# Attention state scan, softmax-weighted layer and routed experts on one core: half slots moved among the slots, product steps and one addition moved in VectorE's order

## The chip, the cores and the metric

The kernel runs on one core of one Trainium2 chip. The metric is the device time in microseconds (us) of one execution; lower is better. A kernel is timed several times, and its median is quoted. One further reading is the profiled execution, of which the trace gives every instruction.

## The reference

Three stages follow each other. Shapes: batch B = 4, heads H = 8, sequence S = 768, head dimension D = 48, so 3072 tokens of 384 numbers; all in float32.

```python
# 1: a linear recurrence over the sequence, per batch and head, with a complex decay a
S_re, S_im = a_re*S_re - a_im*S_im + outer(k[t], v[t]),  a_re*S_im + a_im*S_re
y[t] = q[t] @ S_re
# 2: x is y laid out as (3072, 384)
h = x @ w_in                       # (3072, 1024)
solu = h * softmax(h)
x = layernorm(solu) * g_ln @ w_out # (3072, 384)
# 3: two of eight experts for each token, by noisy logits
out[token] += weight[token, k] * (relu(x[token] @ w1[e]) @ w2[e])   # w1: 384x1024, w2: 1024x384
```

## The kernel before

**First phase, tokens.** Stages 1 and 2 and the routing of stage 3 run in 24 steps n = 4c + b, one for each chunk c of 128 positions (six) and batch b (four). `over_tiles` calls one `body(c, b, n)` for every engine; in it the engines work on different tiles at once: VectorE (DVE) prepares tile n, the matmul engine (PE) works on tile m = n-1 of the recurrence, on i = n-2 of the hidden product (L1624) and on j = n-3 of the second product (L1672). Each engine runs its own list in order, and semaphores join the lists. What is multiplied is split into a high and a low part, so each product of the layers is three matmuls.

In DVE's body the places that matter stand in this order: the low part `zl` (L1343), the maximum (L1369), the product with the softmax (L1388), the addition of a new term to the running state (L1394, semaphore `w_added`), then `weigh` and `k_products` (kp, L1236), the low part `xl` of the new tile (L1412, semaphore `xt_lo`), `q_products` (qp, L1227). Between them lie seven numbered places, `fill(0)` to `fill(6)`. Each call issues as many steps of the cumulative products of the decays (`product_op`, L1112 to L1140) as the table `FILLS` gives for this place: row `FILLS[0]` serves c = 0 and `FILLS[1]` serves c = 1 to 4, with one tuple for each b. The first 45 of 63 steps of a chunk are chain steps (L1112, L1117, L1120 in turn), the other 18 carry steps (four of L1134, then L1137 and L1140). `norm` scales the decays of a later chunk.

PE's list for step n is: transposes of kp (L1554), hidden product (L1624, 24 matmuls, which wait for `xt_lo` of the step before), `a_mm` (L1646, which waits for `zl` and qp), the new state term (L1661), the second product (L1672), L1684, transposes, L1690, the gate logits (L1704, which wait for `w_added` of the tile of this step), transposes of z.

**Second phase, experts.** The routed rows are cut into 31 slots: 25 whole slots of 256 rows and 6 half slots of 128. The tuple `HALF_SLOTS` says which of the 31 are halves; `table_row` maps a slot to its row of the routing table, `give_block` and `units` read the tuple too. A slot s loads `w1` and `w2` of its expert (1.5 MB each, SyncE's queue SP), splits them in high and low (ScalarE, L825 and L830, then DVE, L1241 and L1247), and computes eight blocks f: hidden product (L1563), relu (ScalarE `hh`, L1032), low part (DVE `hl`, L1509), output product (L1764). A half slot needs the same weights and half the matmuls, and it is ordered in another way (`half_slot`; its output product is L1792).

The output is accumulated in memory, so the slots form a chain. `partial(s)` on GpSimd (POOL) gathers the rows of `out` into `prev` (L731) once the rows that slot s-1 scattered have landed (`y_sent`). `give(s)` on DVE adds the slot's product to them (`yo`, L1502), and POOL's `give` scatters them back (L740). DVE carries out `give(s-1)` inside slot s, behind block f = `give_block(s-1)`, or near the start of a half slot: `give_block` is 4 in the slot right behind a half slot, then 3, 2, and 1 from there on. Everything of DVE behind `give` waits with it, the `hl` of the next blocks included.

SP's loop loads, for each s in turn, `mine` of slot s+3 (after `y_sent` of slot s-3) and then the weights of slot s+1.

Of the kernel before, what the change touches and what calls it, by code (L numbers as in the profile page):

```python
# [31 lines left out]
MAXS = NTOK // CAP  # L32
WHOLE, HALVES = 25, 6
SLOTS = WHOLE + HALVES
HALF_SLOTS = (3, 8, 12, 17, 21, 26)
ROWS = (E + 1) * REGION
NG = 3
LINE = 16
# [18 lines left out]
def is_half(s):  # L57

    return s in HALF_SLOTS


def table_row(s):

    return WHOLE + HALF_SLOTS.index(s) if is_half(s) else s - sum(t < s for t in HALF_SLOTS)

# [6 lines left out]
def units_upto(s, step=1):  # L72

    return sum(units(t) for t in range(s, -1, -step))


def give_block(s):

    return max([GIVE] + [4 - (s - t) for t in HALF_SLOTS if t <= s])


def steps(s):

    return sum(2 if is_half(t) else FC for t in range(s))


def wait(eng, sem, value):

    if isinstance(value, int) and value <= 0:
        return  # L90
    eng.wait_ge(sem, value)
# [29 lines left out]
def solu_moe_program(nc, q, k, v, a_re, a_im, w_in, w_out, g_ln, w_gate, w_noise, noise, w1, w2, out):  # L121
# [3 lines left out]
    with ExitStack() as ctx:  # L125
# [246 lines left out]
        def part(t, q):  # L372
            return t[:, :, :, q % 2, :, :].rearrange("p g h x i -> p (g h) (x i)")
# [10 lines left out]
        def mag(q, s_):  # L384

            return cum_part(q, s_) if q < 4 else magnitude[:, s_]

        def spare(h_, g):

            return slice(64 * h_ + D, 64 * h_ + 64), slice(64 * h_ + 16 * g, 64 * h_ + 16 * (g + 1)), g  # L390

        def spread_first(eng, h_):

            t = rcs[0].rearrange("p n h c x i -> p n (h c x i)")
            for from_, to, g in SPARE[NG * h_:NG * (h_ + 1)]:
                eng.dma_start(t[to, NG], t[from_, g]).then_inc(rc_spread, 16)

        SPARE = tuple(spare(h_, g) for h_ in range(2) for g in range(NG))
        FILLS = (((0, 0, 0, 0, 0, 0, 0), (0, 0, 0, 0, 0, 0, 16), (4, 1, 6, 1, 2, 3, 17), (4, 9, 0, 0, 0, 0, 0)),
                 ((6, 1, 9, 1, 2, 0, 3), (12, 1, 3, 1, 2, 1, 0), (8, 1, 2, 1, 3, 0, 4), (2, 0, 0, 0, 0, 0, 0)))  # L400
        assert all(sum(map(sum, x)) == CHAIN + CARRY for x in FILLS)

        def gated(group):
# [11 lines left out]
        def apart(eng, *waits):  # L415


            for s_, x in waits:
                wait(eng, s_, x)
                eng.sem_inc(passed[eng.engine], 1)  # L420
# [339 lines left out]
        def _(act):  # L760
# [282 lines left out]
            def half_slot(s, par, more):  # L1043

                s0, k = steps(s), 2 * HALF_SLOTS.index(s)

# [29 lines left out]
        def _(dve):  # L1076
# [100 lines left out]
            def norm(q):  # L1177
                ar, ai = ars[q // 2 % 2], ais[q // 2 % 2]
                s_ = mag(q, 0)
                dve.wait_ge(sc_done, q + 1)  # L1180
                V.tensor_tensor(part(ar, q), part(ar, q), s_, ALU.mult).then_inc(an_done, 1)
                halves = [t.rearrange("p (g h) x -> p g h x", h=2) for t in (part(ai, q), s_)]
                low, high = ([t[:, :, h_, :] for t in halves] for h_ in range(2))
                V.scalar_tensor_tensor(out=low[0], in0=low[0], scalar=-1.0, in1=low[1], op0=ALU.mult,
                                       op1=ALU.mult).then_inc(an_done, 1)
                V.tensor_tensor(high[0], high[0], high[1], ALU.mult).then_inc(an_done, 1)
# [105 lines left out]
            def body(c, b, n):  # L1292
# [4 lines left out]

                fills = FILLS[c > 0][b] if prep else (0,) * 7
                made = [sum(map(sum, FILLS[c > 0][:b]))]

                def fill(place):

                    for k_ in range(fills[place]):
                        product_op(c + 1, made[0] + k_)
                    made[0] += fills[place]
# [74 lines left out]
                if has(i):  # L1380
                    s0 = 4 * i
                    par = i % 2
                    dve.wait_ge(solu_step, s0 + 1)
                    V.reciprocal(esum[:, 2:3], esum[:, 1:2]).then_inc(solu_step, 1)
                    fill(3)

                    apart(dve, (solu_step, s0 + 2), (rstd_done, 2 * (i - 1)))
                    V.scalar_tensor_tensor(out=z[:], in0=z[:], scalar=esum[:, 2:3],  # L1388
                                           in1=bank[:, 4:6, :].rearrange("p b x -> p (b x)"), op0=ALU.mult,
                                           op1=ALU.mult, accum_out=mv[par][:, 0:1]).then_inc(solu_step, 1)  # L1390
                if B <= m < LIVE:

                    apart(dve, (w_mm, m + 1), (state_step, 3 * (m - B + 1)), (wide_done, 2 * (m - B + 1)))
                    V.tensor_tensor(state[:, m % B].rearrange("p s n e -> p (s n e)"),  # L1394
                                    state[:, m % B].rearrange("p s n e -> p (s n e)"),
                                    bank[:, 6, 0:2 * NP * D], ALU.add).then_inc(w_added, 1)
                fill(4)
                if c == 0 and b == 2:
                    norm(2 * c + 4)
                if b == 3 and c + 2 < C:  # L1400
                    norm(2 * c + 5)
                if b == 3 and prep:
# [22 lines left out]
                if b == 3 and prep:  # L1425
                    newton(2 * c + 2)

            over_tiles(dve, body)


# [119 lines left out]
        def _(pe):  # L1550
# [191 lines left out]
            def expert_hidden(s, par, f):  # L1742
# [3 lines left out]
                if f == 0 and s > 0 and is_half(s - 1):  # L1746
                    pe.wait_ge(row_done, 2 * HALF_SLOTS.index(s - 1) + 1)
                else:
# [29 lines left out]
            def half_turn(s, par, part):  # L1778
                if part == 0:
                    wait(pe, y2_evac, units_upto(s - 2))  # L1780
                pe.wait_ge(row_done, 2 * HALF_SLOTS.index(s) + part + 1)
                for k_ in range(4):
# [99 lines left out]
```

## Time and profile before

| | us |
|---|---|
| median of 3 runs | 1122.89 |
| the three runs | 1119.02, 1122.89, 1128.33 |
| the profiled execution, its own time | 1128.33 |
| its span in the trace | 1126.6 |

The profile covers the execution with 1128.33, the longest of the three; the time around its span is 1.7 us. The page gives busy time by engine, the span in 40 slices, the queues, the chain that ended last and the costliest groups. A row of a timeline reads: start, duration, engine, line, operation, output and inputs, shape, how many merged, and in brackets how long the engine was idle before it and who released it. PEclk is the granted clock of the matmul engine, 1.00 for 2.4 GHz and 0.50 for 1.2 GHz.

### The profile page before, as it was taken

How to read it: one execution, taken by the hardware profiler on the slowest of the kernel's cores; microseconds unless marked ns; L12 is line 12 of the kernel's file. 1: busy time of each engine (PE TensorE's matmuls, PEld its weight loads, DVE VectorE, ACT ScalarE, POOL GpSimd, SP SyncE). 2: the span in 40 equal slices, each digit the busy share in tenths (PEclk: the TensorE clock that was granted, in tenths of full speed). 3: DMA queues.
4: the chain of work that ended last, by engine and by line, in shares of the span. 5: the costliest groups of instructions: out<-in, count | busy, mean ns of one | idle time of the engine just before them, and what ended most of it. 6: DMA issues, size and time to landing. Idle time of an engine off the chain costs nothing.

```text
span 1126.6 us, 20986 instructions
## 1 busy us (share of the span) xinstructions
PE 994.2 (88%) x7460; PEld 924.6 (82%) x7460; DVE 845.6 (75%) x1572; ACT 640.4 (57%) x1081; POOL 423.9 (38%) x389
## 2 busy tenths in 40 slices
PE   0447899999999999999946999999999999999996
PEld 0246798888888888979846999999899999999996
DVE  5799999889899898645554777676766776677672
ACT  6744666856865855635433565565555656455551
POOL 4013133245353443434533334344344434434432
PEclk9868799999999999999967999999999999999998
DMA  9521131241221212221407867776676677667720
GB/s 238 195 94 33 35 102 37 63 93 49 52 92 51 50 37 57 51 57 30 134 15 276 278 220 248 269 249 235 245 262 241 227 265 274 215 244 280 261 72 20
DMA packets 84823, 167.43 MB, mean 149 GB/s; under 512 B 17417, under 2 KB 56544, under 8 KB 84720
## 3 DMA queue, kind: packets, MB, share of 16 engines
q1 hardware_dynamic: 72336, 137.60, 37.9%
q0 software_dynamic: 12288, 28.39, 7.0%
q8 instruction: 60, 0.98, 0.4%
q14 instruction: 43, 0.35, 0.1%
q10 hardware_dynamic: 96, 0.10, 0.0%
HBM read 146.46 MB, written 20.74 MB: 148 GB/s over the span
## 4 chain that ended last, share of the span: by engine, by line
PE 39%; DMA 12%; issue 6%; DVE 4%; ACT 2%; POOL 1%; POOLq 0%; DVEq 0%; another core or an unknown queue 0%; ACTq 0%; SPq 0%
PE bank L1563 12%; PE bank L1764 10%; DMA prev<-out,mine 8%; PE bank L1624 4%; PE bank L1672 4%; DMA out<-yo,mine 3%; PE bank L1554 3%; PE bank L1792 2%; DVE yo L1502 2%; PE bank L1646 1%; PE bank L1684 1%; DVE w1l L1241 1%; ACT z L991 1%; POOL prev L731 0%; POOL out L740 0%
## 5 line engine op out<-in xcount | busy, mean ns | idle before, releaser
L1032 ACT ACTIVATE hh<-bank 128x256 fp32r<-128x256 f32 x200 | 76.8, 384 | 219.9 <-PE bank L1563 210.7
L1563 PE MATMUL bank<-sxh,w1h 128*128 128x256 f32 x600 | 172.2, 287 | 2.1 <-issue 2.1
L1563 PE MATMUL bank<-sxh,w1l 128*128 128x256 f32 x600 | 170.2, 284 | 0.0
L1563 PE MATMUL bank<-sxl,w1h 128*128 128x256 f32 x600 | 169.9, 283 | 0.0
L1509 DVE SCALAR_TENSOR_TENSOR hl<-bank,hh 128x256 fp32r<-128x256 f32 x200 | 84.5, 423 | 91.7 <-ACT hh L1032 85.2
L1764 PE MATMUL bank<-w2h,hh 128*128 128x384 f32 x400 | 136.3, 341 | 5.5 <-DVE hl L1509 5.5
L740 POOL DMA_INDIRECT out<-yo,mine x56 | 67.0, 1197 | 193.4 <-DVE yo L1502 185.8
L1764 PE MATMUL bank<-w2l,hh 128*128 128x384 f32 x400 | 134.9, 337 | 0.0
L1764 PE MATMUL bank<-w2h,hl 128*128 128x384 f32 x400 | 134.8, 337 | 0.0
L1247 DVE TENSOR_TENSOR w2l<-raw,w2h 128x768 fp32r<-128x768 f32 x124 | 117.4, 961 | 20.5 <-ACT w2h L830 20.0
L1241 DVE TENSOR_TENSOR w1l<-raw,w1h 128x1024 fp32r<-128x1024 f32 x93 | 112.4, 1221 | 20.7 <-ACT w1h L825 19.8
L1563 PEld LDWEIGHTS bank<-sxh,w1h 128*128 128x128 f32 x600 | 114.1, 190 | 2.5 <-issue 2.5
L1563 PEld LDWEIGHTS bank<-sxh,w1l 128*128 128x128 f32 x600 | 114.8, 191 | 0.0
L1563 PEld LDWEIGHTS bank<-sxl,w1h 128*128 128x128 f32 x600 | 114.5, 191 | 0.0
L731 POOL DMA_INDIRECT prev<-out,mine x56 | 74.3, 1327 | 101.4 <-DMA out<-yo,mine 84.3
L830 ACT ACTIVATE w2h<-raw 128x768 fp32r<-128x768 f32 x124 | 101.6, 837 | 0.0
L825 ACT ACTIVATE w1h<-raw 128x1024 fp32r<-128x1024 f32 x93 | 96.3, 1051 | 0.0
L668 POOL TENSOR_SCALAR_AFFINE_SELECT at<-at 128x1024 f32<-128x1024 f32 x24 | 28.8, 1201 | 177.7 <-ACT at L939 177.7
L1624 PE MATMUL bank<-wi_hi,xh 112*128 112x512 f32 x192 | 80.5, 419 | 3.0 <-issue 3.0
L1764 PEld LDWEIGHTS bank<-w2h,hh 128*128 128x128 f32 x400 | 76.4, 191 | 7.4 <-DVE hl L1509 3.5
L939 ACT ACTIVATE at<-bank 128x1024 f32<-128x1024 f32 x24 | 24.6, 1023 | 94.6 <-PE bank L1646 94.6
L1624 PE MATMUL bank<-wi_lo,xh 112*128 112x512 f32 x192 | 78.1, 407 | 0.0
(237 smaller groups left out, 2564.1 us busy)
## 6 DMA issues: line engine op xcount, KB each, us to landing
raw<-in_w SPq DMA_DIRECT2D x62, 1536.0 KB
ar<-in_a_re SPq DMA_DIRECT2D x6, 768.0 KB, 4.8
turn<-in_a_im SPq DMA_DIRECT2D x6, 768.0 KB, 6.9
qk<-in_q SPq DMA_DIRECT2D x48, 96.0 KB, 2.4
qk<-in_k SPq DMA_DIRECT2D x48, 96.0 KB, 2.5
out<-wide SPq DMA_DIRECT2D x9, 512.0 KB, 12.3
vt<-in_v SPq DMA_DIRECT2D x24, 192.0 KB, 2.6
xs<-x SPq DMA_DIRECT2D x24, 192.0 KB, 2.6
```

What stands on the lines that cost most here:

```text
L731: nc.gpsimd.indirect_dma_start(prev[par][:, u, :], None, out, bass.IndirectOffsetOnAxis(ap=mine[k][:, u, 0:1], axis=0), bounds_check=NTOK ...
L740: nc.gpsimd.indirect_dma_start(out, bass.IndirectOffsetOnAxis(ap=mine[k][:, u, 0:1], axis=0), yo[par][:, u, :], None, bounds_check=NTOK - ...
L825: nc.scalar.activation(w1h[par][:, cc, :], raw1[par][:, cc, :], ACT.Copy).then_inc(w1_hi, 1)
L830: nc.scalar.activation(w2h[par][:, W2C * j:W2C * (j + 1), :], raw2[par][:, W2C * j:W2C * (j + 1), :], ACT.Copy).then_inc(w2_hi, 1)
L1032: nc.scalar.activation(hh[:, f % NH, :], bank[:, f % 2, 0:CAP], ACT.Relu).then_inc(hh_done, 1)
L1241: V.tensor_tensor(w1l[par][:, cc, :], raw1[par][:, cc, :], w1h[par][:, cc, :].bitcast(F32), ALU.subtract).then_inc(w1_lo, 1)
L1247: V.tensor_tensor(w2l[par][:, cut, :], raw2[par][:, cut, :], w2h[par][:, cut, :].bitcast(F32), ALU.subtract).then_inc(w2_lo, 1)
L1509: V.scalar_tensor_tensor(out=hl[:, f % NH, :], in0=bank[:, f % 2, 0:CAP], scalar=0.0, in1=hh[:, f % NH, :].bitcast(F32), op0=ALU.max, op1= ...
L1563: ins = MM(dst, stationary[a_](cc), moving[b_](cc), start=(n_ == 0), stop=(n_ == len(terms) - 1))
L1624: ins = MM(bank[:, 4 + half, :], (xh, xl)[a_][0:PR, cc, :], (wi_hi, wi_lo)[b_][0:PR, cc, 512 * half:512 * half + 512], start=(k_ % (3 * NP ...
L1672: ins = MM(bank[:, 0, 0:DM], (zh, zl)[a_][:, cc, :], (wo_hi, wo_lo)[b_][:, cc, :], start=(k_ == 0), stop=(k_ == len(x_terms) - 1))
L1764: ins = MM(bank[:, Y_BANK[par] + u, 0:DM], a_[:, f % NH, rows], b_[par][:, f, :], start=(f == 0 and k_ == 0), stop=(f == FC - 1 and k_ == 2))
```

## The change

Three edits:

1. `HALF_SLOTS` goes from (3, 8, 12, 17, 21, 26) to (3, 8, 13, 18, 23, 28). The distances between half slots were 5, 4, 5, 4, 5 and are 5, 5, 5, 5, 5; behind the last half slot came four whole slots and now come two.
2. `FILLS` moves product steps from place 6 (behind `q_products`) to place 5 (between `k_products` and `xl`): nine in c = 0, b = 2; three in b = 0 and four in b = 2 of c = 1 to 4.
3. The addition of the state (L1394) moves behind `fill(4)`, and behind a `norm` that exists in a step where there is no such addition.

```diff
-HALF_SLOTS = (3, 8, 12, 17, 21, 26)
+HALF_SLOTS = (3, 8, 13, 18, 23, 28)
...
-        FILLS = (((0, 0, 0, 0, 0, 0, 0), (0, 0, 0, 0, 0, 0, 16), (4, 1, 6, 1, 2, 3, 17), (4, 9, 0, 0, 0, 0, 0)),
-                 ((6, 1, 9, 1, 2, 0, 3), (12, 1, 3, 1, 2, 1, 0), (8, 1, 2, 1, 3, 0, 4), (2, 0, 0, 0, 0, 0, 0)))
+        FILLS = (((0, 0, 0, 0, 0, 0, 0), (0, 0, 0, 0, 0, 0, 16), (4, 1, 6, 1, 2, 12, 8), (4, 9, 0, 0, 0, 0, 0)),
+                 ((6, 1, 9, 1, 2, 3, 0), (12, 1, 3, 1, 2, 1, 0), (8, 1, 2, 1, 3, 4, 0), (2, 0, 0, 0, 0, 0, 0)))
...
+                fill(4)
+                if c == 0 and b == 2:
+                    norm(2 * c + 4)
                 if B <= m < LIVE:
 
                     apart(dve, (w_mm, m + 1), (state_step, 3 * (m - B + 1)), (wide_done, 2 * (m - B + 1)))
                     V.tensor_tensor(state[:, m % B].rearrange("p s n e -> p (s n e)"),
                                     state[:, m % B].rearrange("p s n e -> p (s n e)"),
                                     bank[:, 6, 0:2 * NP * D], ALU.add).then_inc(w_added, 1)
-                fill(4)
-                if c == 0 and b == 2:
-                    norm(2 * c + 4)
```

## Rows read from the trace of the kernel before

**Rows 1.** Page, part 2: PE's granted clock in the 40 slices of the span.

```profile
PEclk9868799999999999999967999999999999999998
```

**Rows 2.** Windows by stage: bounds, length, busy of PE, PEld, DVE, ACT, POOL, clock, DMA.

```profile
400.00:480.00 80.00, 77.04 (x698) 69.11 (x697) 64.44 (x145) 46.47 (x86) 35.53 (x36) 1.00 0.20 49
...
598.00:1116.00 518.00, 506.41 (x3465) 496.87 (x3466) 359.77 (x507) 283.27 (x465) 201.82 (x164) 0.98 0.68 237
```

**Rows 3.** Waits of PE in the second phase (598 to 1126 us): total, times, longest.

```profile
PE bank L1764 <- DVE hl L1509: 5.5, 5, 1.8
```

**Rows 4.** Windows between the starts of the xg transposes of successive slots.

```profile
692.71:710.28 17.57, 17.57 (x127) 17.54 (x126) 11.73 (x18) 9.55 (x17) 7.33 (x5) 1.00 0.72 257
710.28:729.43 19.15, 18.02 (x127) 17.68 (x126) 13.81 (x21) 10.03 (x17) 8.78 (x8) 1.00 0.71 253
729.43:741.36 11.93, 11.93 (x80) 11.50 (x78) 9.23 (x13) 7.72 (x13) 5.91 (x5) 1.00 0.67 232
741.36:757.01 15.65, 15.40 (x103) 14.70 (x102) 12.50 (x17) 9.68 (x16) 6.15 (x5) 1.00 0.60 211
792.15:807.70 15.55, 13.75 (x80) 13.11 (x79) 11.44 (x16) 8.21 (x14) 7.02 (x6) 0.89 0.62 220
...
952.50:971.88 19.38, 17.24 (x102) 16.34 (x101) 12.39 (x17) 9.77 (x16) 9.61 (x8) 0.91 0.64 225
1007.02:1026.63 19.61, 18.09 (x128) 17.68 (x127) 14.67 (x22) 10.04 (x17) 8.78 (x8) 1.00 0.68 244
```

**Rows 5.** Timeline of DVE: the accumulation yo in slots 7 and 11.

```profile
725.55 1.14 DVE L1502 SCALAR_TENSOR_TENSOR yo<-bank,mine,prev 128x384 f32<-128x384 f32 x2 [1.72 <-DMA prev<-out,mine]
...
792.85 1.14 DVE L1502 SCALAR_TENSOR_TENSOR yo<-bank,mine,prev 128x384 f32<-128x384 f32 x2 [2.82 <-DMA prev<-out,mine]
```

**Rows 6.** Windows of about 3.3 us behind PE's waits in slots 11 and 7.

```profile
796.10:799.40 3.30, 3.30 (x16) 3.30 (x15) 2.15 (x4) 0.10 (x1) 1.14 (x1) 0.50 0.32 119
...
728.40:731.80 3.40, 3.40 (x24) 3.36 (x25) 2.71 (x4) 0.90 (x3) 1.46 (x2) 1.00 0.53 194
```

**Rows 7.** Timeline of DVE in the last slot, slot 30.

```profile
1102.59 1.13 DVE L1502 SCALAR_TENSOR_TENSOR yo<-bank,mine,prev 128x384 f32<-128x384 f32 x2
...
1106.47 0.42 DVE L1509 SCALAR_TENSOR_TENSOR hl<-bank,hh 128x256 fp32r<-128x256 f32 x1 [1.69 <-ACT hh L1032]
...
1116.76 1.14 DVE L1502 SCALAR_TENSOR_TENSOR yo<-bank,mine,prev 128x384 f32<-128x384 f32 x2 [1.41 <-PE bank L1764]
```

**Rows 8.** Windows of half a microsecond: the last one with DMA before 1118 us.

```profile
1112.00:1112.50 0.50, 0.50 (x6) 0.50 (x5) 0.00 (x0) 0.10 (x1) 0.00 (x0) 1.00 0.07 1
```

**Rows 9.** Timeline of DVE, steps 16 and 18: xl, chain steps, carry steps.

```profile
402.62 0.69 DVE L1412 TENSOR_TENSOR xl<-bank,xh 112x512 fp32r<-112x512 f32 x1
...
407.40 0.36 DVE L1112 TENSOR_TENSOR ct<-cum,ar 128x192 f32<-128x192 f32 x1
...
408.47 0.36 DVE L1112 TENSOR_TENSOR ct<-cum,ar 128x192 f32<-128x192 f32 x1
...
439.70 0.69 DVE L1412 TENSOR_TENSOR xl<-bank,xh 112x512 fp32r<-112x512 f32 x1 [0.73 <-ACT xh L997]
...
441.51 1.96 DVE L1134 TENSOR_TENSOR turn<-cum 128x384 f32<-128x384 f32 x4
```

**Rows 10.** Timeline of PE: first matmul of the hidden product behind steps 16 and 18.

```profile
403.61 0.48 PE L1624 MATMUL bank<-wi_hi,xh 112*128 112x512 f32 x1
...
440.96 0.48 PE L1624 MATMUL bank<-wi_hi,xh 112*128 112x512 f32 x1
```

**Rows 11.** Waits of PE from 100 to 560 us: total, times, longest.

```profile
PE bank L1554 <- DVE kp L1236: 13.3, 12, 2.4
```

**Rows 12.** Timeline of step 6: the state addition, the gate logits, the kp transposes.

```profile
188.87 0.54 DVE L1394 TENSOR_TENSOR state<-state,bank 128x384 f32<-128x384 f32 x1
...
189.52 0.81 PE L1704 MATMUL bank<-wg,x2t 128*128 128x16 f32 x6
...
193.06 1.10 PE L1554 MATMUL bank<-ident,kp 128*128 128x128 f32 x8 [1.55 <-DVE kp L1236]
```

## The prediction

> **What bounds the kernel now.** I read the windows by stage first. From 598 to 1116 us, the expert slots, PE is busy for 506.41 of 518 us, DVE for 359.77 [rows 2]: the slots run at PE's pace, and what can be won is PE's 11.6 idle microseconds and what half clock costs. In the first phase PE and DVE are both nearly full; from 400 to 480 us PE is busy 77.04 of 80 and DVE 64.44 [rows 2]. The clock by slice is a full 9 almost throughout the second half and lower at the start and at the seam (the 6 and 7 in the middle) [rows 1].
>
> Next, which wait of PE ends last in the slots. Its list of waits names the low part `hl`, 5.5 us in five waits of 1.8 at most [rows 3]. The page's means hide where they are, so I took windows between the starts of the xg transposes, which mark the slots. A whole slot without a wait takes 17.57 us, the way into a half slot 11.93 and out of it 15.65. Five windows are longer: 19.15 and 19.61 for a whole slot (slots 7 and 25), 15.55 and 19.38 around the half slots 12 and 21 [rows 4], and slot 16, which is of the kind of 7 and 25 and lies near them. Third, DVE's timeline says why `hl` is late: it stands behind `yo`, which waited 1.72 us in slot 7 and 2.82 us in slot 11 for the gather `prev` [rows 5]. So the chain through memory (yo, scatter, gather, yo) is what ends last there. Fourth, the granted clock behind these waits: behind PE's wait in slot 11 it is 0.50 for 3.3 us, behind that in slot 7 it stays 1.00 [rows 6].
>
> **Edit 1, the half slots.** A half slot is short, so the chain falls behind; `give_block` puts `give` at block 4 and takes it forward by one block a slot. In the three slots behind a half slot two successive gives are therefore one block, about 2.1 us, closer than a slot is long: 15.4 us. With a distance of 5 the slot ahead of the next half has its give at block 1 and loses 19.15 - 17.57 = 1.6 us (slot 7) or 19.61 - 17.57 = 2.0 us (slot 25) [rows 4]; I take 1.8 for each of the three (7, 16, 25). With a distance of 4 the half slot arrives one slot earlier, while the give is at block 2, and the chain has about 4 us less: 15.55 - 11.93 = 3.6 us lost around half slot 12, 19.38 - 15.65 = 3.7 around 21 [rows 4]. Of either, about 1.7 us is the stretch of 3.3 to 3.4 us at half clock (half of it is lost) [rows 6]. Before: 3 x 1.8 + 3.6 + 3.7 = 12.7 us. After: the slots 7, 12, 17, 22 and 27 each stand ahead of a half at distance 5: 5 x 1.8 = 9.0 us. Gain 3.7 us. Work and weights of a slot are the same wherever it stands; idle rows skip their transfers as before.
>
> The Trainium skill (TensorE: Matmul & The Clock Gate, HAM oscillation) says that waits for data between bursts of matmuls drop the clock and are paid again in slow matmuls. The trace agrees for slot 11, clock 0.50 behind the wait, and not for slot 7, clock 1.00 [rows 6]. By that rule each of five waits would have its price; that is the first rival below.
>
> **The end, which edit 1 also touches.** The last half slot was four slots from the end and is now two. So `give(29)` in slot 30 goes from block 1 to block 3. Now its yo starts at 1102.59; the `hl` of block 3 is at 1106.47 and yo would follow at about 1106.8, 4.2 us later [rows 7]. The gather for the last slot ends its transfers by 1112.5 [rows 8]; shifted by 4.2 this is 1116.7, and the last yo, which waits for both, starts at 1116.76 on PE's account [rows 7]. The cover of 4.2 us is used up to the last tenth, and the signal behind the last packet comes on top. Bounds: nothing, if the signal is quick, and 4.2 us, the whole shift. The nearest row is the half microsecond in which the traffic ends, so I stay near the low end and take 1.0.
>
> **Edit 2, product steps ahead of xl.** DVE's total is unchanged, and the steps keep their order; `xl` and `q_products` come later, and `zl` stays where it was. PE's hidden product waits for `xl`. Three chain steps take 408.47 - 407.40 = 1.07 us, four carry steps 1.96 us [rows 9]. In step 16 (c = 4, b = 0) `xl` ends at 403.31 and PE starts at 403.61 [rows 9, 10]; the closest that PE follows is about 0.1, so 0.2 us are cover and about 0.85 is a new delay. In step 18, `xl` was idle for 0.73 us, ends at 440.39, and PE starts at 440.96 [rows 9, 10]: 1.96 - 0.73 - 0.47 = 0.76 us. Between there and the end of c = 4 PE has no wait that could absorb it: together 1.6 us. In steps 4 to 14 the same delays, 0.7 to 1.8 us each, meet PE's waits for kp in the step behind: twelve of them, 13.3 us in all, 2.4 at most [rows 11]. kp stands ahead of the moved steps and is not later, so these waits shrink instead: nothing. In step 2 nine steps, some 3.3 us, go ahead of `xl`; PE waits there later for `zl` anyway. I take nothing, with 2 us as the other bound, for the clock was at half in parts of it. If all the cover were gone, eight delays of about 1.3 us would be 10 us; so all of edit 2 lies between 0 and 10. Queued behind the moved `q_products` is SP's load of the next q and k, which has a whole step of 19 us until it is used. No price.
>
> **Edit 3, the state addition.** It goes behind two chain steps (0.7 us), three carry steps (1.5 us) or none. DVE is not idle ahead of it, so nothing is won. PE's gate logits wait for it: in step 6 it ends at 189.41 and PE starts at 189.52 [rows 12], so a delay of 1.5 us reaches PE at once. Behind it PE waits 1.55 us for kp [rows 12], and kp is not later. The cover and the delay are equal within 0.1: 0 to 0.3 us over the five steps where the logits follow at once; I take nothing. Without that cover it would be 2 x 1.5 + 3 x 0.7 = 5.1 us.
>
> **Sum.** -3.7 + 1.0 + 1.6 = -1.1 us. Against the profiled execution that is 1128.33 - 1.1 = 1127.2 (span 1125.5); it was the longest of the three, 5.4 above the median. For the median, 1122.89 - 1.1 = 1121.8 us.
>
> **Rivals.**
>
> *The waits at distance 5 drop the clock too* (slower). Place: slots 7, 12, 17, 22, 27. Price: 1.7 us for each, 8.5 in all: -1.1 + 8.5 = +7.4, 1130.3 us. It outweighs the gain from the third slot on that does so. For it: PE's waits of 1.8 in slot 11 did it. Against: slot 7 did not [rows 6].
>
> *The slots no longer wait at all*: even distances let the chain recover, and all of 12.7 us come back: -12.7 + 2.6 = -10.1, 1112.8 us. For it: only the irregular ones lose 3.6. Against: slots 7 and 25 lose at distance 5 already [rows 4].
>
> *Edit 1 wins nothing*: the longer waits in slots 11 and 21 come from where the weight loads (237 GB/s on average [rows 2]) fall upon the gather, and they move to other slots. Then 0 + 2.6: 1125.5 us.
>
> *The cover in the first phase fails*: PE and DVE take turns as the one that is late, and delays add instead of being absorbed. Half of 10 + 5.1 on top: -1.1 - 1.6 + 7.5 = +4.8, 1127.7 us.
>
> *The first phase pays*: the 0.73 us idle ahead of `xl` is used, no delay reaches PE, the end has its cover: -3.7 - 0.7 = -4.4, 1118.5 us.
>
> **How the numbers follow.** The forecast has 0.45; the clock 0.10, no waits at all 0.08, nothing won 0.12, cover fails 0.12, first phase pays 0.13. The predicted time is 1121.8. The range takes in the forecast, nothing won, the cover failing and the first phase paying, with the spread of the three runs around the median (4 down, 5 up) as a reason not to be narrower: 1115 to 1128. Within 1% is 1111.7 to 1134.1, about what a measurement of this kernel can tell from no change; every case lies inside it, and the outer bounds of the unknown costs reach past it only when they add up. Faster by over 1%: 0.06, within 1%: 0.89, slower by over 1%: 0.05.
>
> **What would show each step right or wrong.** Windows between the xg transposes: all lengths 17.57, 11.93 and 15.65 but for slots 7, 12, 17, 22, 27 with 1.5 to 2.0 more, and none of 3.6 more; the clock at 1.00 from 620 us on. In slot 30 yo at block 3, and the last yo idle for `prev` instead of PE. In steps 16 and 18, the first L1624 about 0.1 us behind `xl` with steps L1112 or L1134 ahead of it; DVE's 0.7 us idle there gone; in steps 4 to 14 the waits for kp shorter by what the hidden product started late. I would be wrong if the end waits more than 2 us for `prev`, if the clock falls in more than one of the five slots, or if DVE is found idle for PE in c = 1 to 3 where it was not.

## The result and the profile after

| | us |
|---|---|
| before, median (19 runs) | 1125.29 (1119.02 to 1129.10) |
| after, median (19 runs) | 1132.55 (1125.47 to 1137.82) |
| ratio after to before | 1.0055, 95% interval 1.0038 to 1.0074 |
| the profiled execution of after, its own time and span | 1130.34, 1128.6 |

The change makes the kernel slower by 0.55%, 6.2 us (4.3 to 8.3). The forecast was -1.1 us. In absolute terms 1132.55 stands against the predicted 1121.8 and lies outside the stated range of 1115 to 1128; 2.4 of these 10.8 us are the kernel before itself, whose median is 1125.29 over 19 runs and was 1122.89 over the three known at the prediction. Differences below are the ratio's distance from 1 times about 1125 us, with its interval. The two profiled executions differ by only 2.0 us, so a trace shows where time goes but not how much it is on average; that is what the medians are for.

The windows by stage and around slot 27 of the changed kernel, to be read as [rows 2, 4]:

```profile
400.00:480.00 80.00, 77.49 (x670) 70.09 (x670) 61.82 (x145) 43.16 (x78) 28.18 (x30) 0.96 0.18 47
600.00:1117.00 517.00, 504.89 (x3465) 495.24 (x3466) 359.79 (x507) 282.97 (x465) 193.19 (x164) 0.98 0.68 238
1037.59:1061.92 24.33, 19.00 (x128) 18.53 (x127) 15.28 (x23) 10.02 (x17) 9.27 (x8) 0.90 0.60 210
1061.92:1074.72 12.80, 12.80 (x79) 12.37 (x78) 8.23 (x12) 7.72 (x13) 4.41 (x4) 0.93 0.52 175
...
1059.90:1063.80 3.90, 3.90 (x15) 3.80 (x16) 2.41 (x3) 0.00 (x0) 1.52 (x2) 0.50 0.37 110
```

From the first xg transposes to those of slot 30 pass 489.9 us (1090.36 - 600.49), before 490.7: in these two executions the slots last equally long, but the time is lost in other places. The third row runs from the transposes for slot 27 to those for half slot 28: 24.33 us where a slot takes 17.57. The slots 7, 12, 17 and 22 lose 1.70, 0.98, 0.62 and 1.13 us in the same trace; slot 27 loses 6.76, and the window behind it another 0.87 (12.80 where it takes 11.93), more than those four together. The last row shows the clock at 0.50 behind the wait, on both sides of the border between the two windows. PE's waits in the second phase, against [rows 3]:

```profile
PE bank L1764 <- DVE hl L1509: 7.9, 7, 4.8
```

One wait of 4.8 us is new. Its surroundings in the timelines of DVE, PE, POOL and SP:

```profile
1057.11 1.14 DVE L1502 SCALAR_TENSOR_TENSOR yo<-bank,mine,prev 128x384 f32<-128x384 f32 x2 [5.39 <-DMA prev<-out,mine]
...
1059.86 0.66 PE L1764 MATMUL bank<-w2h,hh 128*128 128x384 f32 x1 [4.80 <-DVE hl L1509]
...
1039.32 1.20 POOL L740 DMA_INDIRECT out<-yo,mine  x1 [6.74 <-DVE yo L1502]
1040.83 1.13 POOL L740 DMA_INDIRECT out<-yo,mine  x1 [0.31 <-issue]
1048.09 1.59 POOL L731 DMA_INDIRECT prev<-out,mine  x1 [6.13 <-DMA out<-yo,mine]
...
1026.78 0.36 SPq L564 DMA_DIRECT2D mine<-tags  x1
1027.96 0.38 SPq L554 DMA_DIRECT2D raw<-in_w  x1
...
1041.31 0.38 SPq L554 DMA_DIRECT2D raw<-in_w  x1
```

Read from the bottom: SP issues the 1.5 MB of w1 for slot 29 at 1041.31, while POOL is issuing slot 25's scatter (1039.32 to 1041.96). It is the first weight load that has no `mine` ahead of it: slot 30's `mine`, at 1026.78, was the last. POOL then waits 6.13 us behind the scatter's second issue until the rows have landed; in the other 28 waits of this kind in the trace it is 2.0 to 4.4 us, 2.44 in many. The two halves of the scatter part here: the one issued at 1039.32, ahead of the load, lands 2.8 us after its issue, the one issued at 1040.83 lands 6.4 us after it. The gather `prev` of slot 26 is issued that much later, yo in slot 27 waits 5.39 us for it, and PE 4.80. The Trainium skill (DMA: Bandwidth & Descriptors, Issuing engines are not separate DMA queues) says that transfers started by different engines run on the same DMA engines and interleave; the trace agrees: POOL's scatter, with SP's load issued beside it, is waited for 6.13 us and not 2.44.

In the first phase, PE's waits from 100 to 560 us, against [rows 11]:

```profile
PE bank L1624 <- issue: 12.2, 10, 4.3
PE bank L1704 <- issue: 8.5, 6, 3.8
PE bank L1554 <- DVE kp L1236: 6.2, 8, 2.2
```

Waits moved: those for kp went from 13.3 to 6.2 us, and the hidden product and the logits wait instead. All of PE's waits there add up to 28.0 us before and 30.0 after. At the end of the kernel:

```profile
1107.84 1.13 DVE L1502 SCALAR_TENSOR_TENSOR yo<-bank,mine,prev 128x384 f32<-128x384 f32 x2
...
1118.85 1.14 DVE L1502 SCALAR_TENSOR_TENSOR yo<-bank,mine,prev 128x384 f32<-128x384 f32 x2 [2.48 <-DMA prev<-out,mine]
```

The last yo now waits for `prev` and not for PE [rows 7]. From the transposes for slot 30 (1090.36; 1089.34 before) to it are 28.49 us, before 27.42: 1.1 us more.

### The profile page after: what moved, and what is told of

Its sections match the earlier page's. It is cut to its first block, busy times and chain, and to the rows that moved or that the text cites. A ratio compares the mean times of both kernels' runs of the same rounds, so it can differ in the third digit from the quotient of the medians.

```text
span 1128.6 us, 20986 instructions
## 1 busy us (share of the span) xinstructions
PE 992.8 (88%) x7460; PEld 923.3 (82%) x7460; DVE 842.6 (75%) x1572; ACT 639.6 (57%) x1081; POOL 402.6 (36%) x389
## 4 chain that ended last, share of the span: by engine, by line
PE 43%; DMA 10%; issue 6%; DVE 4%; ACT 2%; POOL 1%; POOLq 0%; DVEq 0%; ACTq 0%; SPq 0%
PE bank L1563 13%; PE bank L1764 10%; DMA prev<-out,mine 6%; PE bank L1624 5%; PE bank L1672 4%; PE bank L1554 3%; DMA out<-yo,mine 3%; PE bank L1792 2%; PE bank L1646 2%; DVE yo L1502 2%; PE bank L1684 2%; DVE w1l L1241 1%; ACT z L991 1%; POOL out L740 1%; ACT w1h L825 0%
## 5 line engine op out<-in xcount | busy, mean ns | idle before, releaser
L731 POOL DMA_INDIRECT prev<-out,mine x56 | 70.9, 1267 | 97.4 <-DMA out<-yo,mine 85.9
```

What stands on the lines that cost most here:

```text
L731: nc.gpsimd.indirect_dma_start(prev[par][:, u, :], None, out, bass.IndirectOffsetOnAxis(ap=mine[k][:, u, 0:1], axis=0), bounds_check=NTOK ...
```

## The experiments

Theory A: the loss is slot 27. SP's loop holds back the weights of slot s+1 by the wait of `load_mine(s + 3)`, for the scatter of slot s-3. From s = 28 on there is no `mine` left, and nothing keeps the load off a scatter. Before, that fell on the slots behind half slot 26, which have late gives (blocks 4 and 3); now it falls on slot 27, with its give at block 1. Theory B: the loss is in the first phase, where delays add instead of being absorbed.

### The three edits one by one

Edit 1 alone:

```diff
-HALF_SLOTS = (3, 8, 12, 17, 21, 26)
+HALF_SLOTS = (3, 8, 13, 18, 23, 28)
```

> Only the half slots move; the first phase is that of before. Theory A (the loss is in the last slots: the weight load of slot 29 starts unpaced while slot 25's scatter lands, and slot 27, now a slot with its give at block 1, waits for prev): +3 to +5 us against before, with one wait of PE of 3 to 5 us in slot 27 and the other slots 3 to 6 us cheaper than before together. Theory B (the loss is in the first phase, where delays add instead of being absorbed): -3 us or less, and no long wait in slot 27 beyond chance.

Measured: 1.0052 (1.0029 to 1.0076), +5.8 us. The long wait is there again, 4.70 us, with the load at 1038.29 and the scatter issued from 1036.29 on:

```profile
1038.29 0.38 SPq L554 DMA_DIRECT2D raw<-in_w  x1
...
1045.10 1.55 POOL L731 DMA_INDIRECT prev<-out,mine  x1 [6.16 <-DMA out<-yo,mine]
...
1056.74 0.66 PE L1764 MATMUL bank<-w2h,hh 128*128 128x384 f32 x1 [4.70 <-DVE hl L1509]
```

Edit 2 alone: the `FILLS` table of after in the kernel before.

> Only the product steps move to the place ahead of xl. Theory A: +1 to +2.5 us, what the trace of the changed kernel shows at the seam (600.49 against 598.62). Theory B: +5 us or more.

Measured: 1.0023 (1.0000 to 1.0046), +2.6 us (0 to 5.2).

Edit 3 alone: the addition behind `fill(4)` in the kernel before.

> Only the state addition moves behind the product steps of place 4. Theory A: within 1 us of before; PE's gate logits start later where they follow the addition, and the wait for kp behind them shrinks. Theory B: +2 us or more.

Measured: 0.9985 (0.9959 to 1.0011), -1.7 us (-4.6 to +1.2), no difference that is clear.

Edits 2 and 3 together: after, with the old half slots.

> The changed kernel with the old half slots: edits 2 and 3 together. From the two alone (+2.6 and -1.7): +0.9 us against before; by the prediction: +1.6 us. If the two edits hurt each other in the first phase (the cover of one used up by the other): +4 us or more.

Measured: 1.0001 (0.9976 to 1.0026), +0.1 us (-2.7 to +2.9). So the first phase costs 2.9 us at most and by the median nothing, and edit 1, with 5.8 us alone, carries the 6.2. Theory B falls.

### Holding the last loads back

```diff
                 if s + 3 < SLOTS:
                     load_mine(s + 3, (s + 3) % NM)
+                else:
+                    apart(sp, (y_sent, 16 * units_upto(s - NM + 3)))
                 load_w1(s + 1)
                 load_w2(s + 1)
```

> The changed kernel, with SyncE's queue waiting for the scatter of slots 25 and 26 before it loads the weights of slots 29 and 30, as the load of mine makes it wait in all slots before. Theory A: the wait of 4.8 us in slot 27 goes down to the 0.4 to 1.0 us of slots 12, 17 and 22, and the clock stays full: 5 to 8 us less than the changed kernel, so 0 to 2 us under before. Theory B: no change against the changed kernel, +6 us against before.

Measured: 1.0002 (0.9981 to 1.0023), +0.2 us against before, so 6.0 us less than the changed kernel (the intervals of the two, -2.1 to +2.6 and 4.3 to 8.3, do not meet). Slot 27 in its trace; the two added lines make every later line number two higher:

```profile
1042.65 0.38 SPq L554 DMA_DIRECT2D raw<-in_w  x1
...
1037.53 1.20 POOL L742 DMA_INDIRECT out<-yo,mine  x1 [7.68 <-DVE yo L1504]
1039.03 1.14 POOL L742 DMA_INDIRECT out<-yo,mine  x1 [0.31 <-issue]
1042.60 1.08 POOL L733 DMA_INDIRECT prev<-out,mine  x1 [2.43 <-DMA out<-yo,mine]
...
1053.73 0.41 PE L1766 MATMUL bank<-w2h,hh 128*128 128x384 f32 x1 [0.44 <-DVE hl L1511]
```

The load starts 5.1 us behind the scatter's first issue (1037.53), where in the changed kernel it was 2.0; POOL waits 2.43 us for the scatter, whose two halves each land 2.7 to 2.8 us after their issue, and PE waits 0.44 where it waited 4.80. The window of slot 27 (1034.84 to 1054.87) is still 2.5 us longer than 17.57, for PE waits 1.48 us near its start as well, at 1038.21; but the clock stays at 1.00.

The same with edit 1 alone, and with the kernel before:

> Edit 1 alone with the paced weight loads of slots 29 and 30; the first phase is that of before. This is the term of the prediction's sum by itself: -3.7 for the even distances and +1.0 for the end, so -2.7 us against before. If the even distances win nothing and only the unpaced load was wrong with edit 1: 0 to +1 us. If the pacing was not what took the loss away: +5 us, as edit 1 alone had.

Measured: 0.9994 (0.9975 to 1.0013), -0.7 us (-2.8 to +1.5).

> The kernel before with the same two paced loads. If the unpaced load only hurts where it meets a slot with its give at block 1 (slots 27 of the changed kernel), before gains nothing: within 1.5 us. If it hurts wherever it stands, 3 us or more less than before.

Measured: 1.0016 (0.9994 to 1.0038), +1.8 us (-0.7 to +4.3). Before gains nothing that is clear of noise. Its trace shows why nothing was to be won: the unpaced loads hold up the scatters there too, but the rows are needed later.

```profile
1040.39 0.38 SPq L554 DMA_DIRECT2D raw<-in_w  x1
...
1043.09 1.02 POOL L740 DMA_INDIRECT out<-yo,mine  x1 [7.14 <-DVE yo L1502]
...
1050.95 1.68 POOL L731 DMA_INDIRECT prev<-out,mine  x1 [4.93 <-DMA out<-yo,mine]
...
1056.17 0.38 SPq L554 DMA_DIRECT2D raw<-in_w  x1
...
1065.17 1.02 POOL L731 DMA_INDIRECT prev<-out,mine  x1 [5.83 <-DMA out<-yo,mine]
...
1072.72 1.14 DVE L1502 SCALAR_TENSOR_TENSOR yo<-bank,mine,prev 128x384 f32<-128x384 f32 x2 [0.96 <-DMA prev<-out,mine]
```

POOL waits 4.93 and 5.83 us for the scatters of slots 25 and 26. But the give of slot 26 stands at block 4 and its yo does not wait, that of slot 27 stands at block 3 and waits 0.96 us, and PE does not wait for it in the slots 26 to 29.

### The cause everywhere, and the give of slot 26 later

The kernel before, with the weights ahead of `mine` in SP's order:

```diff
-                if s + 3 < SLOTS:
-                    load_mine(s + 3, (s + 3) % NM)
                 load_w1(s + 1)
                 load_w2(s + 1)
+                if s + 3 < SLOTS:
+                    load_mine(s + 3, (s + 3) % NM)
```

> The kernel before, with SyncE's queue issuing the weights of slot s+1 ahead of mine of slot s+3 instead of behind it, so no weight load is held back by the scatter of slot s-3. If the order of the queue is what keeps weight loads off the scatter (theory A), every slot now meets what slot 27 of the changed kernel met: the gather prev is issued 5 to 6 us behind the scatter instead of 2.4, and the tight slots 7, 11/12, 16, 21 and 25 lose 4 to 7 us each: 15 to 25 us more than before. If slot 27's wait had another cause: within 3 us of before.

Measured: 1.0310 (1.0279 to 1.0341; four runs), +34.9 us, more than expected. The expectation's total did not follow from its own price: five places at 4 to 7 us are 20 to 35. In the trace these five lose 4 to 8 us each more than before, 30 together. Its windows around slots 7 and 25:

```profile
712.42:737.81 25.39, 18.99 (x127) 18.52 (x126) 15.53 (x23) 10.03 (x17) 9.16 (x8) 0.95 0.53 180
1034.04:1058.70 24.66, 19.62 (x128) 19.21 (x126) 14.70 (x22) 10.02 (x17) 8.74 (x8) 0.93 0.56 183
```

The scatter of slot 5 and the gather for slot 6, which yo in slot 7 needs, in its timelines of POOL and SP:

```profile
715.44 1.20 POOL L740 DMA_INDIRECT out<-yo,mine  x1 [4.64 <-DVE yo L1502]
...
717.43 0.38 SPq L554 DMA_DIRECT2D raw<-in_w  x1
...
724.33 1.47 POOL L731 DMA_INDIRECT prev<-out,mine  x1 [6.25 <-DMA out<-yo,mine]
```

And its waits of PE in the second phase, against [rows 3]:

```profile
PE bank L1764 <- DVE hl L1509: 20.6, 8, 4.6
...
PE bank L1792 <- DVE hl L1528: 8.8, 2, 4.4
```

The slots 7 and 25, 19.15 and 19.61 us before [rows 4], now lose 7.8 and 7.1 us, what slot 27 lost in the changed kernel. PE's waits for `hl` grow by 22.0 us (20.6 + 8.8 against 5.5 and 1.9 for the half slots before); the clock at half behind most of them costs more. The load at 717.43 stands 2.0 us behind the scatter's first issue, as in slot 27. So the cause of slot 27 is the order of SP's queue, and it can be made at will.

Edit 1 alone, unpaced, with slot 26's give at block 3:

```diff
-    return max([GIVE] + [4 - (s - t) for t in HALF_SLOTS if t <= s])
+    return max([3 if s == 26 else GIVE] + [4 - (s - t) for t in HALF_SLOTS if t <= s])
```

> Edit 1 alone, loads unpaced, but the give of slot 26 stands behind block 3 of slot 27 instead of block 1 (4.2 us later). If the late scatter hurts only because slot 27's give stands early (theory A), PE's wait of 4.7 us there goes to under 1 us and the clock stays full: 4 to 7 us less than edit 1 alone, within 2 us of before. If the wait has to do with the half slot 28 itself, the later give makes it longer: as edit 1 alone or slower.

Measured: 1.0032 (1.0012 to 1.0052), +3.6 us (1.4 to 5.9): 2.2 less than edit 1 alone, not 4 to 7, and the two intervals overlap.

```profile
1062.14 1.14 DVE L1502 SCALAR_TENSOR_TENSOR yo<-bank,mine,prev 128x384 f32<-128x384 f32 x2 [1.02 <-DMA prev<-out,mine]
...
1064.12 1.20 POOL L740 DMA_INDIRECT out<-yo,mine  x1 [4.61 <-DVE yo L1502]
...
1073.43 1.35 POOL L731 DMA_INDIRECT prev<-out,mine  x1 [6.80 <-DMA out<-yo,mine]
...
1064.65 0.38 SPq L554 DMA_DIRECT2D raw<-in_w  x1
...
1081.56 0.69 PE L1792 MATMUL bank<-w2h,hh 128*128 128x384 f32 x1 [2.88 <-DVE hl L1528]
```

In slot 27 yo waits only 1.02 us. But its scatter, now later, meets the second unpaced load, w1 of slot 30 at 1064.65, and POOL waits 6.80 us for it; the half slot 28 waits 2.88 us. In the changed kernel that load came later behind the scatter of slot 26 and cost nothing:

```profile
1059.08 1.21 POOL L740 DMA_INDIRECT out<-yo,mine  x1 [5.48 <-DVE yo L1502]
...
1062.55 0.38 SPq L554 DMA_DIRECT2D raw<-in_w  x1
...
1064.17 1.04 POOL L731 DMA_INDIRECT prev<-out,mine  x1 [2.44 <-DMA out<-yo,mine]
```

The first wait was taken away and a second made. A late give hides a late scatter only if the next one is free.

### Even distances without the end

```diff
-HALF_SLOTS = (3, 8, 12, 17, 21, 26)
+HALF_SLOTS = (1, 6, 11, 16, 21, 26)
```

> Half slots 1, 6, 11, 16, 21, 26: all distances are 5 as in the changed kernel, but the last half slot stays where it was, so slot 27 keeps its give at block 4 and slot 30 at block 1; loads unpaced. By the prediction's price of the distances: -3.7 us against before and no wait over 2 us in slots 25 to 30. If even distances win nothing: within 1 us of before.

Measured: 0.9990 (0.9970 to 1.0009), -1.1 us (-3.4 to +1.0). No wait over 2 us in the last slots, but not the -3.7 us expected either.

The same with edit 3:

> Half slots 1, 6, 11, 16, 21, 26 and edit 3: the two variants that were fastest by their medians. If their differences (-1.1 and -1.7) are real and add up: -2.8 us against before. If they are noise: within 1 us.

Measured: 0.9976 (0.9959 to 0.9994), -2.7 us (-4.6 to -0.7). It is the only one whose interval lies under 1, and it was picked as the best of several, so its true gain may be smaller.

That kernel with `5 - (s - t)` in `give_block`:

> Half slots 1, 6, 11, 16, 21, 26 and edit 3 as in the fastest variant so far (-2.7 us against before), and behind a half slot the gives stand at blocks 5, 4, 3, 2 instead of 4, 3, 2, 1. If the loss of the tight slots is only that the chain through memory has about 2 us too little there (theory A), 2.1 us more take the 1.4 to 2.9 us of slots 5, 10, 15, 20 and 25 away: 5 to 8 us less, so -8 to -11 us against before. If the give ahead of the half slot then comes too late for the half slot's own give (18.4 us apart before, 16.3 then), the loss only moves there, as with the late give of slot 26: within 2 us of the variant without.

Measured: 1.0021 (1.0006 to 1.0037), +2.4 us, so 5 more than without: neither branch named that. Two waits of its trace:

```profile
680.05 0.41 PE L1764 MATMUL bank<-w2h,hh 128*128 128x384 f32 x1 [1.79 <-DVE hl L1509]
...
958.62 0.51 PE L1792 MATMUL bank<-w2h,hh 128*128 128x384 f32 x1 [2.04 <-DVE hl L1528]
```

The second is in half slot 21, as the expectation's other branch had it; the first, in slot 5, is not. Why slots 5 and 15 still lose 2 us with a later give was not settled: the whole row of gives moved, and with `y_sent` the weight loads moved too.

## Why the prediction was wrong

**The step that failed.** "After: the slots 7, 12, 17, 22 and 27 each stand ahead of a half at distance 5: 5 x 1.8 = 9.0 us." Four of them did what it says, or better. Slot 27 lost 6.8 us in the trace of after and 7.4 with edit 1 alone, and 0.9 and 1.7 more behind it, instead of 1.8. The step took a slot's price to hang on its distance from the half slots only ("Work and weights of a slot are the same wherever it stands"). It hangs on SP's queue too, whose pacing ends with the last `mine`. The prediction had SP's loop and the chain through memory before it, but did not lay one on the other for the last three slots. The trace of before had the slow scatters too (POOL's waits of 4.93 and 5.83 us), but gives at blocks 4 and 3 hid them from PE. Shown: the wait is in both traces with the unpaced load, gone with it paced (6.0 us less), and can be made in the other tight slots (+34.9 us).

**A term that was mis-sized.** The 3.6 and 3.7 us for the distances of 4 came from one execution. In four more traces the half slots are the old ones; the two windows in the trace of edit 2 alone are:

```profile
798.05:810.46 12.41, 12.21 (x79) 11.58 (x78) 10.53 (x15) 8.20 (x14) 6.50 (x6) 1.00 0.65 233
956.11:975.50 19.39, 17.27 (x102) 16.36 (x101) 12.40 (x17) 9.78 (x16) 9.11 (x7) 0.91 0.64 228
```

in that of edit 3 alone:

```profile
790.01:802.59 12.58, 12.20 (x80) 11.56 (x79) 10.72 (x15) 8.21 (x14) 6.48 (x6) 1.00 0.63 222
947.87:965.07 17.20, 15.69 (x102) 14.78 (x101) 12.34 (x17) 9.79 (x16) 8.08 (x7) 1.00 0.64 219
```

in that of both:

```profile
793.02:805.47 12.45, 12.22 (x80) 11.58 (x79) 10.57 (x15) 8.22 (x14) 6.50 (x6) 1.00 0.65 233
950.37:966.60 16.23, 15.67 (x103) 14.76 (x102) 12.31 (x17) 9.79 (x16) 9.12 (x7) 1.00 0.68 231
```

and in that of before with the paced loads:

```profile
793.40:805.59 12.19, 12.19 (x79) 11.55 (x78) 10.33 (x15) 8.21 (x14) 6.46 (x6) 1.00 0.65 232
950.66:967.02 16.36, 15.68 (x102) 14.78 (x101) 12.34 (x17) 9.78 (x16) 9.17 (x7) 1.00 0.69 237
```

Against 11.93 and 15.65 us without a wait these lose 0.5, 0.6, 0.5 and 0.3 in the first place and 3.7, 1.6, 0.6 and 0.7 in the second; with the profile before (3.6, 3.7) the mean of both together is 3.2 us, not 7.3. The large ones are those in which the clock fell behind the wait (0.89 and 0.91 of the window). So a distance of 4 costs about what one of 5 costs, and evening them out gains about 1 us, if anything: edit 1 with paced loads measured -0.7 (-2.8 to +1.5), the variant that ends at 26 -1.1 (-3.4 to +1.0).

**The end.** +1.0 was forecast; 1.1 us more between the transposes for slot 30 and the last yo, which waits for `prev` as described. In the four other traces with the half slot at 28 it is 0.5 to 1.2 us. The term was right in size and mechanism, though it was chosen between bounds of 0 and 4.2, and the sign that the prediction set against itself, a wait of over 2 us for `prev`, did come: 2.48 us, which took the place of the 1.41 us for PE.

**Edit 2.** +1.6 was forecast; alone it measured +2.6 (0 to 5.2), together with edit 3 +0.1 (-2.7 to +2.9). The direction of single waits was right: the waits for kp shrank and those of the hidden product grew. In step 18 the hidden product starts 0.1 us behind `xl`, with the idle time ahead of `xl` filled:

```profile
444.81 0.68 DVE L1412 TENSOR_TENSOR xl<-bank,xh 112x512 fp32r<-112x512 f32 x1
...
445.59 0.47 PE L1624 MATMUL bank<-wi_hi,xh 112*128 112x512 f32 x1 [0.81 <-issue]
```

Step 16 shows no such thing: `xl` ends at 405.18 and the hidden product starts at 406.06, for PE ran at half clock there (0.50 from 404 to 408 us) and was still at the kp transposes. From 400 to 480 us the mean clock was 0.96, before 1.00; such losses were not in the sum. In all, PE waited 2.0 us more. The seam, 598.62 before and 600.49 after, is no measure of it: in traces with the first phase of before the first xg transpose starts anywhere from 596.18 to 603.99. The size is open between 0 and 5 us.

**Edit 3.** Nothing was forecast; -1.7 (-4.6 to +1.2). Consistent, and neither gain nor loss is shown.

**The rivals.** The clock rival named five waits that each drop it; in the trace of after it fell in slot 27 alone, where the wait was 4.8 us, and the other four stayed full (waits of 0.4 to 1.0 us). Read as a rule for every wait, what the prediction took for this rival did not hold. The rival that edit 1 wins nothing because weight loads meet the gather named the right actors, the loads and the small transfers, and put them in the wrong places; its 1125.5 us had no price for a wait of 4.8 us. The first-phase rival (1127.7) put +7.5 us on edits 2 and 3, which together measured 2.9 at most: refuted. That the slots wait no more is refuted too: in every trace with these half slots at least three of the slots 7, 12, 17 and 22 wait. That the first phase pays (-0.7) can't be told from +0.1.

**Sum of what was found.** Edit 1: about -1 for the distances, +1 for the end, +6 for slot 27, and the first phase about 0: +6, where 6.2 was measured. Only the 6 is clear of noise; the other terms are each within their intervals of nothing.

## What to carry to other kernels

A wait that stands in a queue for another reason (here for a buffer of indices) can be what keeps large transfers off small urgent ones behind it; look for the iterations in which that wait is missing, and see whether the tightest step of a dependency chain falls on them. When a schedule is moved by a slot, lay every queue's timeline over the new tight places, the last iterations above all. A price that contains a clock drop, taken from one trace, is a draw and not a mean: look at the same window in several executions before multiplying it.

## What the runs showed of the hardware

**A large load beside a small scatter.** What counts is when a load of 1.5 MB (w1 or w2) is issued on SP's queue, reckoned from the first of the two issues of a whole slot's scatter. POOL's wait behind the second issue, where the profile puts it down to the scatter, over all fourteen traces:

| load issued | POOL waits, us | cases |
|---|---|---|
| 2.6 to 2.7 us ahead | 3.4 to 6.5 | 11 |
| 0.5 us behind | 6.0 to 7.0 | 6 |
| 2.0 us behind | 6.1 to 6.3 | 6 |
| 3.5 us behind | 2.4 to 2.5 | 5 |
| 4.1 to 4.3 us behind | 2.5 to 3.2 | 4 |
| 5.1 to 5.2 us behind | 2.4 to 2.6 | 3 |

A load issued 2.0 us behind falls into the second issue, one issued 3.5 us behind comes 0.8 us after its end (1059.08 and 1062.55 in the trace of after): there the price is gone. What the small transfer waits for inside the DMA engines, no run here tells.

**Waits and the clock.** Of PE's waits of 0.95 us and more in the slots of the fourteen traces, none of the 29 up to 1.79 us was followed by half clock, 9 of the 14 from 1.80 to 2.88 us were, for 3.4 us each, and all five of 4.3 us and more were, for 3.4 or 6.8 us. Between 1.8 and 2.9 us the same wait was paid again in one execution and not in another.
